# Head logits moved between scores and transposes, head 4's raw load ahead of v, another order of the first loads

## The reference, cut to what matters

```python
q_n, k_n, c_n = (t / (norm(t) + 1e-06) for t in (q, k, centroids))
q_assign = argmax(einsum('bhsd,hcd->bhsc', q_n, c_n))
k_assign = argmax(einsum('bhsd,hcd->bhsc', k_n, c_n))
mask = q_assign[:, :, :, None] == k_assign[:, :, None, :]
scores = where(mask, (q @ k.T) / sqrt(64), -1e9)
attn = exp(scores - max(scores)); attn = attn / (sum(attn) + 1e-9)
x = attn @ v                                      # tokens 1536 x 512
x = (((x @ w1) * (x @ w2)) @ w3) @ w_out          # 512 -> 1024 -> 512
h = x @ w_in; x = (h * clip(h + 3, 0, 6) / 6) @ w_out2   # 512 -> 2048 -> 512
```

## Time and profile before

| | us |
|---|---|
| median of 3 runs | 713.5 |
| the profiled execution | 715.35 |
| its span in the profile | 713.5 |
| PE busy | 705.0 |
| DVE, POOL, ACT busy | 496.1, 446.5, 390.9 |

### The profile page before, as it was taken

The page is one execution under the profiler, slowest core; times in us unless marked ns, Lnnn a source line. Parts: engine busy times, 40 slices in busy tenths (PEclk is TensorE's granted clock), DMA queues, the critical chain, the costliest instruction groups (busy, mean ns, idle before and its releaser), DMA issues.

```text
span 713.5 us, 11831 instructions
## 1 busy us (share of the span) xinstructions
PE 705.0 (99%) x4017; PEld 607.4 (85%) x4017; DVE 496.1 (70%) x754; ACT 390.9 (55%) x808; POOL 446.5 (63%) x455
## 2 busy tenths in 40 slices
PE   8998999999999999999999999999999999999998
PEld 6787777776767767999999999999988889998886
DVE  6237787877878786677986779888865547874221
ACT  6315565656656575454554445477754447775333
POOL 5953553453354475996969969788557769753221
PEclk9999999999999999999999999999999999999999
DMA  8647765665565413211002110012212233221212
GB/s 294 188 105 201 185 124 133 162 162 139 142 168 125 111 23 71 71 65 55 15 16 86 64 60 1 30 60 89 75 47 73 74 102 120 74 76 60 69 35 90
DMA packets 41772, 68.50 MB, mean 96 GB/s; under 512 B 10224, under 2 KB 17904, under 8 KB 41712
## 3 DMA queue, kind: packets, MB, share of 16 engines
q1 hardware_dynamic: 36048, 64.81, 32.2%
q10 hardware_dynamic: 5664, 2.93, 1.4%
HBM read 44.07 MB, written 3.19 MB: 66 GB/s over the span
## 4 chain that ended last, share of the span: by engine, by line
PE 93%; issue 2%; DVE 2%; ACT 1%; POOL 1%; DMA 1%; SPq 0%; POOLq 0%
PE ps L1377 21%; PE ps L1379 21%; PE ps L1378 21%; PE ps L1503 9%; PE ps L1489 8%; PE ps L1477 5%; PE ps L1479 4%; PE ps L1446 1%; DMA wo_raw<-in_wo 1%; DVE g_lo L1295 1%; ACT probs L799 0%; PE ps L1463 0%; PE ps L1408 0%; PE ps L1411 0%; DVE neg_max L1159 0%
## 5 line engine op out<-in xcount | busy, mean ns | idle before, releaser
L634 POOL TENSOR_TENSOR b_lo<-stage,b_hi 128x512 fp32r<-128x512 f32 x94 | 111.9, 1191 | 101.3 <-ACT b_hi L882 101.1
L1295 DVE TENSOR_TENSOR g_lo<-gate,g_hi 128x384 fp32r<-128x384 f32 x96 | 83.6, 878 | 64.9 <-ACT g_hi L971 64.8
L799 ACT ACTIVATE probs<-ps,neg_max 128x768 f32<-128x768 f32 x96 | 86.8, 904 | 51.4 <-DVE neg_max L1159 50.6
L1159 DVE TENSOR_REDUCE neg_max<-ps 128x1 f32<-128x768 f32 x96 | 91.2, 952 | 25.1 <-PE ps L1479 24.9
L971 ACT CAST g_hi<-gate 128x384 fp32r<-128x384 f32 x96 | 49.2, 514 | 90.4 <-PE ps L1379 90.4
L1489 PE MATMUL ps<-ident,probs 128*128 128x128 f32 x576 | 77.6, 275 | 0.0
L1489 PEld LDWEIGHTS ps<-ident,probs 128*128 128x128 f32 x576 | 66.1, 140 | 13.4 <-ACT probs L799 7.2
L1220 DVE COPY probs_t<-ps 128x512 f32<-128x512 f32 x96 | 63.7, 679 | 17.3 <-PE ps L1489 17.1
L591 POOL TENSOR_TENSOR x_lo<-x_raw,x_hi 128x384 fp32r<-128x384 f32 x15 | 15.2, 1016 | 96.7 <-PE ps L1489 64.4
L1180 DVE TENSOR_TENSOR sum_lo<-sum_raw,sum_hi 128x768 fp32r<-128x768 f32 x64 | 65.2, 1021 | 14.5 <-ACT sum_hi L858 14.3
L1379 PE MATMUL ps<-b_hi,g_lo 128*128 128x512 f32 x192 | 74.8, 389 | 0.0
(11 more groups left out here) (129 smaller groups left out, 1846.7 us busy)
## 6 DMA issues: line engine op xcount, KB each, us to landing
stage<-in_wio SPq DMA_DIRECT2D x64, 256.0 KB, 2.6
qk_ops<-qk_split SPq DMA_DIRECT2D x32, 384.0 KB, 5.8
stage<-in_w SPq DMA_DIRECT2D x46, 256.0 KB, 3.1
qk_raw<-in_qk SPq DMA_DIRECT2D x16, 384.0 KB, 5.2
qk_ops<-qk_split SPq DMA_DIRECT2D x32, 192.0 KB, 5.7
v_raw<-in_v SPq DMA_DIRECT2D x16, 192.0 KB, 2.6
recip_all<-recip_rows SPq DMA_DIRECT2D x32, 96.0 KB, 3.1
out<-out_sb ACTq DMA_DIRECT2D x11, 256.0 KB, 2.2
```

The lines of the kernel that those rows point to most:

```text
L634: nc.gpsimd.tensor_tensor(b_lo[n % 2][:, cols], stage[n % 2][:, cols], b_hi[n % 2][:, cols].bitcast(F32), ALU.subtract).then_inc(s_lo[half ...
L799: nc.scalar.activation(probs[g % PROBS][:].rearrange("p (a b) -> p a b", a=2), scores[g % 2], ACT.Exp, bias=neg_max[:, g:g + 1], scale=1.0 ...
L1159: nc.vector.tensor_reduce(neg_max[:, g:g + 1], scores[g % 2], AX.XY, ALU.max, negate=True).then_inc(s_max, 1)
L1295: nc.vector.tensor_tensor(g_lo[i][:], hidden(q, c, f)[0][:], g_hi[i][:].bitcast(F32), ALU.subtract).then_inc(s_glo, 1)
```

## The change

Four edits. (1) `logits(u+4)` stands in unit u, for u from 0 to 11, behind score(s+7) and ahead of transposes(s+4); before, the same logits stood at the head of the next unit, behind transposes(s+4). The ring order and ACT's copy (ahead of exp(s+7), behind exp(s+6)) move with it. (2) load_raw(4) goes out ahead of load_v(0..3) and the gate blocks. (3) SP's first loads are wo 0, wo 1, rests 0 and 1, centroids, wo 2; ACT's own queue issues the two pieces, ahead of all its work. (4) ACT takes the square root behind wo_high(1) and ahead of rest_high(0); DVE takes wo_low(0) ahead of the centroids' square and wo_low(1) between their sum and the steps behind the root.

```diff
@@ ring_order
-        if u and head(u + 3):
-            uses.append(("logits", u + 3))
         if u:
             uses += fills(s - 1)
...
-            uses += fills(s + 2) + fills(s + 3) + fills(s + 4)
+            uses += fills(s + 2) + fills(s + 3)
+        if head(u + 4):
+            uses.append(("logits", u + 4))
+        if u < UNITS:
+            uses += fills(s + 4)
@@ SP
-            sp.dma_start(cent_raw[:], cent).then_inc(s_cent, 16)
-            load_piece(0)
-            load_wo(0)
-            load_piece(1)
-            load_wo(1)
+            load_wo(0, 1)
             load_rest(0)
             load_rest(1)
+            sp.dma_start(cent_raw[:], cent).then_inc(s_cent, 16)
             load_wo(2, 3)
...
             load_mask(1)
+            load_raw(4)
             for n in range(4):
                 load_v(n)
...
-                if n + 2 < HEADS:
+                if n >= 3 and n + 2 < HEADS:
                     load_raw(n + 2)
@@ ACT
-            act.wait_ge(s_cent_sq, 1)
-            nc.scalar.activation(cs[1][:], cs[0][:], ACT.Sqrt).then_inc(s_sqrt, 1)
+            for n in range(2):
+                act.dma_start(stage[n][:, PIECE], w3[n][:, PIECE]).then_inc(s_piece[n], 16)
             piece_high(0)
             wo_high(0)
             piece_high(1)
             wo_high(1)
+            act.wait_ge(s_cent_sq, 1)
+            nc.scalar.activation(cs[1][:], cs[0][:], ACT.Sqrt).then_inc(s_sqrt, 1)
             rest_high(0)
...
-                if u and head(u + 3):
-                    rows_of_logits(u + 3)
...
+                if head(u + 4):
+                    rows_of_logits(u + 4)
                 group_copies(s + 4)
@@ DVE
+            wo_low(0)
             dve.wait_ge(s_cent, 16)
             step(nc.vector.tensor_tensor(cent_sq[:], cent_raw[:], cent_raw[:], ALU.mult))
             own.wait()
             nc.vector.tensor_reduce(cs[0][:], cent_sq[:], AX.X, ALU.add).then_inc(s_cent_sq, 1)
+            wo_low(1)
...
-            for k in range(F1T):
+            for k in range(2, F1T):
                 wo_low(k)
@@ PE
-                if u and head(u + 3):
-                    logits(u + 3)
...
                 if u < UNITS - 1:
                     score(s + 7)
+                if head(u + 4):
+                    logits(u + 4)
                 transposes(s + 4)
```

More of the change, by code:

```diff
@@ L445, in load_wo @@
                     sp.dma_start(wo_raw[:, k, :], wo[:, k * DM:(k + 1) * DM]).then_inc(s_wo_in[k], 16)
-            def load_piece(n):
-                sp.dma_start(stage[n][:, PIECE], w3[n][:, PIECE]).then_inc(s_piece[n], 16)
             def load_rest(n):
                 sp.dma_start(stage[n][:, REST], w3[n][:, REST]).then_inc(s_stage[0][n], 16)
-            sp.dma_start(cent_raw[:], cent).then_inc(s_cent, 16)
-            load_piece(0)
-            load_wo(0)
-            load_piece(1)
-            load_wo(1)
+            load_wo(0, 1)
             load_rest(0)
             load_rest(1)
+            sp.dma_start(cent_raw[:], cent).then_inc(s_cent, 16)
             load_wo(2, 3)
```

## The result

| | before | after |
|---|---|---|
| median of 5 runs each, us | 713.72 (713.37 to 715.64) | 719.4 (717.23 to 720.35) |
| the profiled execution | 715.35 | 717.23 |
| its span | 713.5 | 715.4 |

The ratio is 1.0067, 95% interval [1.0044, 1.0091]: 5 us slower, where 2.6 us faster was forecast. The profiled execution after is the quickest of the five. Its mean granted clock is 0.998; the other four have 0.998 to 0.995.

What follows compares the result with a forecast made beforehand. PE was taken as the bound, busy 705.0 of 713.5 us. Terms -1.8 (head 4's stall), -1.0 (boundaries), -0.3 (SP behind the stall), +0.5 (front) gave -2.6: median 710.9 us, range 709.7 to 713.0.

Steps and rivals of the forecast that it cites:

- part 4: Front, new load order and ACT/DVE order: a loss of 0.5 us, between a gain of 0.4 and a loss of 1.8.
- I weighed another: Front, ACT's table load: the skill's drain of about 1.38 us beside it would cost about 1.4 us more; trace spoke against.
- My upper bound for the front, 1.8: Front: largest loss in us, if the centroids land only with wo 2 at 9.08.
- Part 1: End of unit 0: loading head 4 earlier removes PE's whole stall of 1.76 us, bounds 1.4 and 1.8.
- Part 2: PE's order at 12 unit boundaries: 0.08 us less each, 1.0 us in all, bounds 0 and 1.2.
- Part 3: First score of head 3, behind SP's late mask loads: 0.3 us gained, bounds 0 and 0.4.
- The second rival: Front: late centroids or a longer table switch on ACT and DVE cost about 1.8 us; 712.2 us, chance 0.15.
- The third: Rival, front: gains 0.4 us, as w_out's tiles lead and ACT had idled; 710.0 us, chance 0.12.
- The fourth: Rival, unit 0: head 4's stall stays, by a late load, exp(7) or bank copies; 712.7 us, chance 0.06.
- The fifth: Rival, 12 units: ACT's logits copy delays exp(s+7) by x, costing 12 (x - 0.4) us; 715.7 at x = 0.8; chance 0.07.

Runs made afterwards that it cites:

- e3: Changed kernel, but POOL's subtractions of the rests wait behind DVE's centroid scalings: 714.49 us, ratio 1.0007 to the kernel before.
- e8: Changed kernel with DVE's two small products in pointer-scalar form and the centroid scalings moved to ACT behind wo_high(3): 713.25 us, ratio 0.9986 to the kernel before.
- e11: Kernel before, plus eight unused row reductions on DVE ahead of the third w_out subtraction: 720.97 us, ratio 1.0092.
- e12: Kernel before, plus five unused row reductions on DVE ahead of the third w_out subtraction: 718.08 us, ratio 1.0054.
- e5: Kernel before with only the logits' new place and head 4's load ahead of v, second measurement: 712.69 us, ratio 0.9976.
- e9: Kernel before with only the logits' new place, head 4's load left where it was: 713.87 us, ratio 1.0001.
- e1: Kernel before with only the logits' new place and head 4's load ahead of v, first measurement: 713.18 us, ratio 0.9983.
- e2: Kernel before with only the front's new load order and new order on ACT and DVE, attention unchanged: 719.82 us, ratio 1.008.
- e10: Kernel before with attention's edits, pieces on ACT's queue, centroids loaded first, pointer-scalar products and scalings on ACT: 713.05 us, ratio 0.9981.

## Why the prediction was wrong

**The step that failed is part 4, its sentence "1.6 us of small steps end at 10.3. wo_low(2) is queued behind them on DVE and ends at 11.0".** The order and the waits in it were right, and the arrivals even better than I took them: the centroids were there by 6.4 (I had 7.5), and the first pass of tile 2 came 0.46 earlier. What failed was that I took the duration of each step from the earlier trace rows, where POOL was idle but for one subtraction (4.02 to 4.74), and moved the chain into a stretch in which POOL works. The steps to the end of the scalings took 12.80 - 8.12 = 4.7 us; e3, with POOL idle, has 9.74 - 8.16 = 1.6, my number. wo_low(2) ended at 13.40 (PE went on at 13.45) instead of 11.0. The same step failed a second time further on: part 4 stops at wo_low(2), and wo_low(7), which it never prices, took 4.62 us beside POOL instead of 1.78 and ended at 22.53 instead of 16.92. That PE waited for both is in the trace, and e3 and e8, which keep the order and free DVE of POOL in the chain, have waits of 0.4 and 0.5 us for tile 2 and none over 0.1 us for a later wo_lo. That POOL stretches wo_low(7) itself is read from the rows and the same growth elsewhere; no run tested it by itself. It ends 0.55 us behind the end of POOL's fourth instruction (21.98), and why it didn't get in behind an earlier one stays open.

The trace of before held the warning. Timelines of DVE and of POOL before: the same subtraction that takes 0.69 alone takes 1.23 beside POOL.

```profile
11.68 1.23 DVE L1100 TENSOR_TENSOR wo_lo<-wo_raw,wo_hi 128x512 fp32r<-128x512 f32 x1 [0.61 <-ACT wo_hi L808]
```
```profile
11.07 2.99 POOL L550 TENSOR_TENSOR b_lo<-stage,b_hi 128x512 fp32r<-128x512 f32 x2 [1.64 <-ACT b_hi L546]
```

The Trainium skill states the rule, on its page SBUF — State Buffer, section "SBUF: two separate sides": DVE and GpSimd share a pair of ports as an exclusive lock, held for a whole instruction, and of DVE's instructions those with two SBUF inputs or in a two-port mode need it. The traces agree: a product of 128 numbers has taken 0.63 to 0.66, which is about one POOL instruction (1.44 / 2 = 0.72), and the pointer-scalar form 0.22. This was the rule that spoke against the change, and I weighed another.

**The half clock was in no term.** It held PE up by 1.6 us on the way, but the wait for wo_lo 7 would have taken them anyhow, so the failed step is DVE's and not this. e11 and e12 show that it comes with a wait of this kind whatever the cause. The Trainium skill, TensorE: Matmul & The Clock Gate, section "HAM oscillation — how this bites in real kernels", describes the same for waits on a transfer: the engine starts its next block at half clock. The windows here agree (0.50 for two microseconds and parts of two more), but for the first 0.8 us behind the changed kernel's wait, which are still at 1.00. My upper bound for the front, 1.8, was an arrival bound; the front cost 5.0 in the profiled execution.

**Part 1 was right**: 1.79 us (5.03 - 3.24), predicted 1.76 to 1.8; POOL began head 4's scaling at 61.49, predicted before 63.

**Part 2 had the sign and the wrong size.** Predicted 0.08 a boundary. Timeline of PE, units 3 and 4, against the earlier trace rows: the intervals are 0.46, 0.56 and 0.63, a sum of 1.65 against 1.67. The third was to be 0.57; transposes behind logits take 0.88 and not 0.82.

```profile
111.39 0.52 PE L1480 MATMUL ps<-qk_ops 80*128 80x384 f32 x2
111.85 0.63 PE L1447 MATMUL ps<-qk_raw,cent_t 128*32 128x256 f32 x6
112.41 0.88 PE L1490 MATMUL ps<-ident,probs 128*128 128x128 f32 x6
113.04 0.59 PE L1478 MATMUL ps<-qk_ops 128*128 128x384 f32 x2
```

Over attention PE gained 0.8 behind head 4, some 0.05 a unit. Of that 0.25 came in one unit (+2.99 to +2.74), where e11, with the old order, gained 0.19 too. Where the rest arises, beyond the 0.02 of the boundary, I did not find.

**Part 3 is not settled.** The 0.4 at the head of unit 2 stayed in the changed kernel (85.71 to 86.66 is 0.95) and is gone in e5, but also in e9, where head 4's load was not moved. So it doesn't hang on edit 2; what it does hang on wasn't tested.

**The second rival** named a slower chain on ACT and DVE. The chain was slower, but not by the late centroids or the table drain that it named; neither happened. The table load ended at 7.80 and the root began at 7.81. Timeline of ACT:

```profile
6.52 1.28 ACT L828 ACT_TABLE_LOAD   x1
7.81 0.20 ACT L828 ACTIVATE cs<-cs 128x1 f32<-128x1 f32 x1
```

So the 1.38 us of drain that the Trainium skill (ScalarE: Activation LUTs, "What ACT_TABLE_LOAD costs") puts beside a load do not show behind this one, nor ahead of it (the cast before it ended at 6.49). **The third** was half right: the loads gained 0.4 and DVE lost them. **The fourth** fell (no wait at 69.92). **The fifth** fell as reckoned: the copy of the logits (112.54, 0.37) and then exp, with score(s+9) on time, x = 0.

**The sum, moved to a median, would have been off as well.** Parts 1 to 3 and no front were to bring 3.1 us. The profiled e5 shows 3.8; the medians of e1 and e5 show 1.1 and 1.6. The profiled execution of before had the longest stall of head 4 of four executions: with the same attention code PE waited 1.7 us there, 1.0 in e2, 0.4 in e11 and 1.5 in e12. From SP's issue of the load to POOL's start it is 8.9, 8.5, 8.1 and 8.9 us. A stall that is the rest of a landing time differs from execution to execution, and one profile gives one sample; and that execution stood 1.85 us above the median, which I took for a constant.

**Still open.** The medians differ by 5.7 us and the two profiled executions by 1.9. Before's stands 1.6 above its median and after's 2.2 below its own. The changed kernel's two runs with a mean clock of 0.995 are among its longest (720.35, 719.56). By that mean they lost 3.6 us of full clock (0.005 x 715, an estimate), twice as much as the profiled one, and where, and whether a wait for DVE covered it, no profile shows. Such runs exist without the long wait too: e3 at 0.998 took 716.16 and 719.74 where its other ten took 713.75 to 715.19, and e9 at 0.995 and 0.998 took 717.07 and 716.73 where its others took 714.29 at most. So the front's DVE chain is shown as the cause of the 5 us, and the last microsecond or so between a profile and a median is not explained.

## What to carry to other kernels

When a chain is moved, take its durations from a stretch in which the other engines do what they will do at the new place; for DVE that means a look at POOL's timeline first, and two-operand steps on 128x1 columns are worth turning into pointer-scalar ones. Follow the moved chain to its last instruction, not to the first that PE waits for: here the last one set the loss. A long wait of PE in dense work can halve the clock behind it, and that costs nothing where a later wait would have taken the time anyhow, as it did here. A gain read off one stall of one execution is one sample of a landing time.

## What was not expected of the hardware

- DVE beside POOL: a 128x1 product of two SBUF columns 0.16 us alone, 0.63 to 0.66 beside a POOL subtraction; two 128x64 scalings 0.42 alone and 2.54 beside two, though they take a pointer scalar; a 128x512 subtraction 0.69 alone and up to 4.62 under five POOL instructions. A 128x1 reciprocal (0.16 at 9.23 in e8) and a 128x1 pointer-scalar operation (0.22) do not grow.
- The clock: behind PE waits of 3.9, 3.5 and 2.5 us in the fold it falls to 0.50 (1.2 GHz), with passes of 1.05 us instead of 0.62. At the start of the fold passes of 1.05 us or more occur behind waits of 0.78 us (e10), 0.25 (the changed kernel, 1.28) and none (e9, 1.22), and no clock is on record there. Other waits of 0.4 to 1.8 us had full speed behind them.
- Logits between scores and transposes: the transposes behind them take 0.88 us for six and not 0.82.
